# Reordering a few vector, scalar and cast steps in the attention stage of a fused attention / gated MLP / routed attention kernel

## The chip, the cores and the metric

The kernel runs on one core of one Trainium2 chip. The metric is the device time of one execution in microseconds, lower is better; of several executions the median counts. The profile shows the granted clock of TensorE and the span from the first to the last instruction; the device time of an execution is a little longer than its span.

## The reference

Three parts follow each other, for 4 batches of 576 tokens:

```
# 1. windowed causal attention, 8 heads of 64
scores = q @ k.T / 8 + alibi_bias            # key at most 127 behind the query, none ahead
attn   = exp(scores - max);  attn /= sum(attn) + 1e-9
x      = heads side by side of (attn @ v)     # 576 x 512
# 2. gated MLP with a spatial matrix
h = relu(x @ w_in);  u, v = halves of h       # w_in is 512 x 1024
v_n = layer norm of v
gated = u * (w_spatial @ v_n + b_spatial);  x = gated @ w_out
# 3. four attention experts (q, k, v of 64), causal, top 2 of 4 by a gate, summed
```

Only the first part's schedule is touched by the change. Its arithmetic stays as it is.

## The kernel before

The program is written engine by engine: each engine has one instruction stream in program order, and every hand-over is a semaphore. No planner orders the work; the order is the order of the calls in `row(b, ...)` of each engine. `row` is called for batches 0 to 3; in batch 0 `first` is true, and the weights are rounded there beside the attention.

Products that need more than the fast matmul format's precision are made of three matmuls: an operand is split into a rounded part ("hi") and what the rounding lost ("lo"). For w_in, ScalarE makes hi (`high_w_in`, L665 to L668) and VectorE makes lo (`low_w_in`, L989 to L993), one 128x512 block (half, k) at a time, in batch 0 only. Half 1 is the v half, which `v_product` uses first.

The first stage handles a batch in 20 groups g = 0 to 19. A group is two heads of a tile of 128 queries (the last tile has 64 queries, and there two heads share one square). Ten steps m = 0 to 9 of two groups each drive the loops of all engines. A group passes through:

- TensorE `scores1` (L1373 to L1400): q times k into PSUM, two groups at a time.
- VectorE `bias1` (L931 to L945): adds the bias and writes to `ring` in SBUF, with the minimum of the negated row, two instructions (one for each head) of 128x256.
- VectorE `join1` (L947 to L954), called a minimum below: the elementwise minimum of the two key blocks of a row, which turns two blocks of 128 keys into one. A query sees each of the two blocks at complementary positions only.
- ScalarE `exp1` (L644 to L654): the exponential with the row's sum, one instruction and one read of the sum for each head; it waits for the join of its own group.
- VectorE `reciprocal1` (L956 to L963): adds the epsilon to the sums and takes the reciprocal, two small instructions; it waits for the exponentials of its own group. The title of the change calls this step "sums".
- GpSimd `scale1` (L533 to L540): scales the two squares by the reciprocals; it waits for `reciprocal1`.
- TensorE `transpose1` (L1436 to L1442): transposes the scaled squares into PSUM; it waits for `scale1`.
- ScalarE `copy_pt1` (L690 to L698): copies the transposed squares of both groups of a step to `pt` in SBUF (in steps 0 and 1 of the first group only).
- VectorE `copy_pt1_second` (L1017 to L1033): from step 2 on, multiplies this copy by a triangular mask of ones into a second plane of `pt` (L1030, the "masked product"); in steps 0 and 1 it copies the second group's squares (L1025).
- TensorE `values1` (L1463 to L1491): times v. Its first matmuls use the plane of `copy_pt1`; after the first four of them it waits for `copy_pt1_second`, whose plane the difference of two v tiles (`v_step`) is multiplied with.
- ScalarE `high_x`, VectorE `low_x`: the rounded x and the rest, once for each tile.

TensorE's order in a step is: scores of a later step, the two transposes of this step, half of a `v_product` (x times the v half of w_in, six matmuls of 512 columns), `values1` of this step. Beside the diff, these places matter for following it:

```
646    i = G1[g][0];  if i: act.wait_ge(s1_cb, joined1(b, g))   # exp waits for the join
960    dve.wait_ge(s1_ex, U1 * b + us[-1][0] + 1)               # reciprocal waits for the exps
1085   elif m < ND1 - 3:       # steps 4, 5, 6 (and 3): bias, reciprocal1(b, 2 * m + 3), join,
1094       copy_pt1_second(m)  # ... then the masked product, bias, join, reciprocal
```

The order of VectorE in step 5 is thus: bias 14, reciprocal 13, join 14, masked product, bias 15, join 15, reciprocal 14. The change does not touch it. The SyncE queue only issues loads and stores; the change moves none of them.

Of the kernel before, what the change touches and what calls it, by code (L numbers as in the profile page):

```python
# [130 lines left out]
def build(nc, qT, kT, v, w_in, wsT, bsp, woT, wcat, wo, out):  # L131
    ctx = ExitStack()
    with ctx:
# [42 lines left out]
        at = region(4 * NT * H * D)  # L176
# [4 lines left out]
        at = region(max(4 * SLOTS1 * 2 * P, 4 * KT * CW))  # L181
# [4 lines left out]
        at = region(4 * P3_SLOTS * S)  # L186
# [5 lines left out]
        at = region(4 * 2 * 512)  # L192
        pt = sb("pt", [P, 2, 512], F32, at)
        pt_hi = sb("pt_hi", [P, 2, 512], F32R, at)
        at = region(8 * KT * S)
# [9 lines left out]
        at = region(8 * NT * DM)  # L205
# [4 lines left out]
        at = region(4 * 4 * DM)  # L210
# [432 lines left out]
        def _(act):  # L643
            def exp1(b, g):  # L644

                i = G1[g][0]
                if i:
                    act.wait_ge(s1_cb, joined1(b, g))
                for u, h in units1(g):
                    x = ring[:, u % SLOTS1, 0:P]  # L650
                    if i == 0:
                        act.wait_ge(s1_bi, U1 * b + u + 1)
                    nc.scalar.activation(x, x, ACT.Exp, bias=neg1[:, u % SLOTS1:u % SLOTS1 + 1], scale=-1.0,  # L653
                                         accum_out=sum1[:, i % 2, h:h + 1]).then_inc(s1_ex, 1)  # L654
# [34 lines left out]
            def row(b, first, more):  # L689
# [48 lines left out]
                for m in range(ND1):  # L738
                    if m % 2 == 0 and m >= 2:
                        high_x(m // 2 - 1)  # L740
                    if m == 0 and not first:
                        copy_pt1(0)
                        exp1(b, 4)
                        copy_out(b - 1, NT - 1)
                    elif m == 2:
                        copy_pt1(2)
                        for g in (6, 7, 8):
                            exp1(b, g)
                    else:
                        if 2 * m + 3 < NG1 - 1:  # L750
                            exp1(b, 2 * m + 3)
                        copy_pt1(m)
                        if 2 * m + 4 < NG1 and m != 1:
                            exp1(b, 2 * m + 4)
                    if m == ND1 - 3:
                        exp1(b, NG1 - 1)
                    if first and m % 2 and m < ND1 - 1:
                        negate_v(m // 2)
                    for half, at in W_IN_AT.items():
                        for k in range(KT):  # L760
                            if first and at[k] == m:
                                high_w_in(half, k)
                    n = m - first
                    if n % 2 and 3 <= n < ND1 - 1:
                        relu_v((n - 3) // 2)
                    if first:
                        for t in WS_AT.get(m, ()):
                            high_w_spatial(t)
# [161 lines left out]
        def _(dve):  # L930
            def bias1(b, g):  # L931

                qb = ORDER1[G1[g][0]]
                w, c0 = width1(qb), (P if qb == 0 else 0)
                m = g // 2
                at = w * (g % 4 if together(b, m) else g % 2)
                dve.wait_ge(s1_sc, ND1 * b + (m | 1 if together(b, m) else m) + 1)
                for n, (u, h) in enumerate(units1(g)):
                    if qb < NT - 1:
                        scores, table = bank[:, s1_banks(b, g // 2)[n], at:at + w], bias[:, h, c0:c0 + w]  # L940
                    else:
                        scores, table = bank[:, S1_BANKS[g % 2], w * (m % 2):w * (m % 2) + w], bias_last[:, h // 2, :]
                    nc.vector.tensor_tensor_reduce(out=ring[:, u % SLOTS1, 0:w], in0=scores, in1=table, scale=-SCALE,  # L943
                                                   scalar=3.0e38, op0=ALU.add, op1=ALU.min,
                                                   accum_out=neg1[:, u % SLOTS1:u % SLOTS1 + 1]).then_inc(s1_bi, 1)  # L945

            def join1(b, g):  # L947

                if g >= NG1 or G1[g][0] == 0:
                    return  # L950
                n = P if G1[g][0] < NT - 1 else LAST
                dve.wait_ge(s1_bi, U1 * b + units1(g)[-1][0] + 1)
                x = ring[:, slots1(g), :]
                nc.vector.tensor_tensor(x[:, :, 0:n], x[:, :, 0:n], x[:, :, P:P + n], ALU.min).then_inc(s1_cb, 1)  # L954

            def reciprocal1(b, g):  # L956

                us = units1(g)
                at = (slice(0, P), G1[g][0] % 2, slice(us[0][1], us[-1][1] + 1))
                dve.wait_ge(s1_ex, U1 * b + us[-1][0] + 1)  # L960
                nc.vector.tensor_scalar(den1[at], sum1[at], EPS_SUM, None, ALU.add).then_inc(s1_dn, 1)
                dve.wait_ge(s1_dn, NG1 * b + g + 1)
                nc.vector.reciprocal(r1[at], den1[at]).then_inc(s1_rc, 1)  # L963
# [52 lines left out]
            def row(b, first, more):  # L1016
                def copy_pt1_second(m):  # L1017
                    n = 2 * columns1(2 * m)
                    if m:
                        dve.wait_ge(s1_pv, NG1 * b + 2 * m)  # L1020
                    if m < 2:
                        if first:
                            return
                        dve.wait_ge(s1_t, NG1 * b + 2 * m + 2)
                        nc.vector.tensor_copy(pt[:, 0, 2 * P:4 * P], bank[:, 3, 0:2 * P]).then_inc(s1_h2, 1)  # L1025
                        return
                    if m == 2 and first:
                        dve.wait_ge(s_diag, 2)
                    dve.wait_ge(s1_h, ND1 * b + m + 1)
                    nc.vector.tensor_tensor(pt[:, 1, 0:n].rearrange("p (h r) -> p h r", h=4),  # L1030
                                            pt[:, 0, 0:n].rearrange("p (h r) -> p h r", h=4),
                                            diag[:, 0:n // 4].unsqueeze(1).to_broadcast([P, 4, n // 4]), ALU.mult
                                            ).then_inc(s1_h2, 1)  # L1033
# [28 lines left out]
                for m in range(ND1):  # L1062
                    if m % 2 == 0 and m >= 2:
                        low_x(m // 2 - 1)
                    if m == 0 and not first:
                        copy_pt1_second(0)
                        join1(b, 5)
                        reciprocal1(b, 3)
                        reciprocal1(b, 4)
                    elif m == 1:  # L1070
                        copy_pt1_second(1)
                        reciprocal1(b, 5)
                        bias1(b, 6)
                        bias1(b, 7)
                        join1(b, 6)
                    elif m == 2:
                        copy_pt1_second(2)
                        join1(b, 7)
                        bias1(b, 8)
                        reciprocal1(b, 6)  # L1080
                        bias1(b, 9)
                        reciprocal1(b, 7)
                        join1(b, 8)
                        join1(b, 9)
                    elif m < ND1 - 3:
                        bias1(b, 2 * m + 4)
                        if m == 3:
                            reciprocal1(b, 8)
                        else:
                            reciprocal1(b, 2 * m + 3)  # L1090
                        join1(b, 2 * m + 4)
                        if m == 3:
                            reciprocal1(b, 9)
                        copy_pt1_second(m)
                        bias1(b, 2 * m + 5)
                        join1(b, 2 * m + 5)
                        reciprocal1(b, 2 * m + 4)
                    elif m == ND1 - 3:
                        bias1(b, NG1 - 2)
                        bias1(b, NG1 - 1)  # L1100
                        reciprocal1(b, NG1 - 3)
                        join1(b, NG1 - 2)
                        join1(b, NG1 - 1)
                        copy_pt1_second(m)
                        reciprocal1(b, NG1 - 2)
                        reciprocal1(b, NG1 - 1)
                    else:
                        copy_pt1_second(m)
                    for half, at in W_IN_AT.items():
                        for k in range(KT):  # L1110
                            if first and at[k] == m and half:
                                low_w_in(half, k)
# [665 lines left out]
```

## Time and profile before

| what | value |
|---|---|
| median of 3 runs | 488.56 us (488.44 to 489.31) |
| the profiled execution's own time | 489.27 us |
| its span | 487.4 us |
| mean granted TensorE clock | 0.996 |
| TensorE matmul busy | 475.3 us (98%) |
| VectorE busy | 317.8 us (65%) |
| ScalarE busy | 272.9 us (56%) |
| GpSimd busy | 202.9 us (42%) |

The first stage of batch 0 lies at about 4 to 48 us of the span, that of batch 1 at about 144 to 180, of batch 2 at 257 to 293, of batch 3 at 371 to 406. Between them lie the matmuls of parts 2 and 3. A busy row is the share of the span in which the engine had an instruction in work; for TensorE matmuls overlap, so that small stalls hardly show in its busy time. They show as a bracket at the row behind the stall: how long the engine sat idle, and what released it.

### The profile page before, as it was taken

The numbers are of one execution on the slowest core, as the hardware profiler recorded it, in microseconds if no ns is written. First come the engines' busy times: TensorE is split into PE (matmuls) and PEld (weight loads), VectorE is DVE, ScalarE is ACT, GpSimd is POOL, SyncE is SP. The second block draws the span as 40 slices with busy tenths as digits, with TensorE's granted clock in tenths as the row PEclk, the third lists the DMA queues.
The fourth block names the chain that finished last, engine by engine and source line by source line (L and its number), as shares of the span: only waits on it lengthen the run. The fifth ranks groups of instructions, "written<-read, shape, count | busy, mean of one in ns | idle before, by whom it ended". The sixth has DMA issues, their size and how long they took to land.

```text
span 487.4 us, 10761 instructions
## 1 busy us (share of the span) xinstructions
PE 475.3 (98%) x3858; PEld 408.5 (84%) x3858; DVE 317.8 (65%) x1247; ACT 272.9 (56%) x827; POOL 202.9 (42%) x373
## 2 busy tenths in 40 slices
PE   8799999999999999999999999999999999999996
PEld 5577998999776789999876689999877679999974
DVE  7886775367778855337778855436777875235783
ACT  6776572346676644245766745334776663335663
POOL 4361614523434418742244525760343443461431
PEclk9899999999999999999999999999999999999999
DMA  7919420004110081002311073002301000000111
GB/s 230 326 64 245 179 86 1 1 1 135 46 33 23 13 240 42 1 0 53 107 34 44 1 196 98 1 1 48 101 32 56 0 1 2 2 1 12 38 45 54
DMA packets 33512, 31.64 MB, mean 65 GB/s; under 512 B 6002, under 2 KB 24434, under 8 KB 33460
## 3 DMA queue, kind: packets, MB, share of 16 engines
q1 hardware_dynamic: 33460, 30.97, 21.2%
q8 instruction: 30, 0.49, 0.4%
q14 instruction: 22, 0.18, 0.1%
HBM read 23.88 MB, written 4.72 MB: 59 GB/s over the span
## 4 chain that ended last, share of the span: by engine, by line
PE 66%; DVE 17%; ACT 11%; issue 4%; POOL 1%; DVEq 0%
PE bank L1412 14%; PE bank L1414 14%; PE bank L1413 14%; ACT p L830 7%; PE bank L1399 5%; PE bank L1483 5%; DVE ring L943 4%; PE bank L1441 3%; DVE p L1194 2%; PE bank L1690 2%; PE bank L1668 2%; PE bank L1418 2%; DVE ring L954 2%; PE bank L1419 1%; DVE pt L1030 1%
## 5 line engine op out<-in xcount | busy, mean ns | idle before, releaser
L539 POOL TENSOR_SCALAR ring<-ring,r 128x128 f32<-128x128 f32 x144 | 60.2, 430 | 86.1 <-DVE r L963 85.8
L625 POOL TENSOR_SCALAR p<-p,r,wgt 128x128 f32<-128x128 f32 (+3 forms) x64 | 38.3, 610 | 93.3 <-DVE wgt_last L1241 50.0
L653 ACT ACTIVATE ring<-ring,neg 128x128 f32<-128x128 f32 x144 | 56.7, 396 | 21.3 <-DVE ring L954 18.1
L830 ACT ACTIVATE p<-p,neg 128x128 f32<-128x128 f32 (+4 forms) x72 | 41.6, 579 | 29.6 <-DVE neg L1194 29.6
L943 DVE CUSTOM_DVE_ANT_0 ring<-bank,bias 128x256 f32<-128x256 f32 (+1 forms) x128 | 43.5, 384 | 2.3 <-PE bank L1399 2.0
L589 POOL TENSOR_TENSOR g_lo<-uT,g_hi 128x288 fp32r<-128x288 f32 x32 | 25.2, 814 | 36.4 <-ACT g_hi L796 20.4
L1412 PE MATMUL bank<-g_hi,w_c_hi 128*128 128x288 f32 x128 | 38.6, 301 | 0.2
L1412 PE MATMUL bank<-x_hi,w_in_hi 128*128 128x288 f32 x128 | 38.2, 298 | 0.0
L1412 PE MATMUL bank<-w_spatial_hi,vn_hi 128*128 128x288 f32 x128 | 37.8, 295 | 0.0
L1414 PE MATMUL bank<-x_hi,w_in_lo 128*128 128x288 f32 x128 | 37.7, 295 | 0.0
L1414 PE MATMUL bank<-w_spatial_hi,vn_lo 128*128 128x288 f32 x128 | 37.7, 294 | 0.0
L1413 PE MATMUL bank<-w_spatial_lo,vn_hi 128*128 128x288 f32 x128 | 37.7, 294 | 0.0
L1413 PE MATMUL bank<-x_lo,w_in_hi 128*128 128x288 f32 x128 | 37.7, 294 | 0.0
L1414 PE MATMUL bank<-g_hi,w_c_lo 128*128 128x288 f32 x128 | 37.7, 294 | 0.0
L1413 PE MATMUL bank<-g_lo,w_c_hi 128*128 128x288 f32 x128 | 37.5, 293 | 0.0
L1399 PE MATMUL bank<-k,q 64*128 64x256 f32 (+2 forms) x320 | 36.8, 367 | 0.0
L1194 DVE CUSTOM_DVE_ANT_0 p<-bank,causal_masks 128x128 f32<-128x128 f32 (+4 forms) x72 | 34.3, 513 | 1.6 <-PE bank L1653 1.4
L1483 PE MATMUL bank<-pt,v_in 128*64 128x128 f32 (+1 forms) x384 | 33.0, 274 | 0.6 <-ACT pt L695 0.6
L796 ACT CAST g_hi<-uT 128x288 fp32r<-128x288 f32 x32 | 12.9, 432 | 35.7 <-DVE uT L1173 35.7
L1483 PEld LDWEIGHTS bank<-pt,v_in 128*64 128x64 f32 x384 | 20.5, 137 | 14.1 <-issue 12.2
L1399 PEld LDWEIGHTS bank<-k,q 64*128 64x128 f32 (+1 forms) x320 | 26.1, 182 | 6.7 <-issue 4.1
L1173 DVE TENSOR_TENSOR uT<-bank,uT 128x288 f32<-128x288 f32 x32 | 13.5, 454 | 27.7 <-PE bank L1596 27.7
(193 smaller groups left out, 1449.0 us busy)
## 6 DMA issues: line engine op xcount, KB each, us to landing
v_in<-v SPq DMA_DIRECT2D x16, 256.0 KB, 4.0
out<-o_sb SPq DMA_DIRECT2D x16, 256.0 KB, 2.0
q<-qT SPq DMA_DIRECT2D x15, 256.0 KB, 4.6
k<-kT SPq DMA_DIRECT2D x15, 256.0 KB, 5.1
v_minus_v_of_tile_above<-v SPq DMA_DIRECT2D x9, 256.0 KB, 3.8
w_in_raw<-w_in SPq DMA_DIRECT2D x4, 512.0 KB, 6.2
w_cat_raw<-wcat SPq DMA_DIRECT2D x1, 1544.0 KB, 6.8
w_spatial_raw<-wsT SPq DMA_DIRECT2D x1, 1152.0 KB, 9.3
```

The lines of the kernel that those rows point to most:

```text
L539: last = nc.gpsimd.tensor_scalar(p, p, r1[:, i % 2, h:h + 1], 0.0, ALU.mult, ALU.add)
L589: nc.gpsimd.tensor_tensor(g_lo[:, dt, c], uT[:, dt, c], g_hi[:, dt, c].bitcast(F32), ALU.subtract).then_inc(s2_gl, 1)
L625: nc.gpsimd.tensor_scalar(p, p, r3[:, i % 2, e:e + 1], by, ALU.mult, ALU.mult).then_inc(s3_sd, 1)
L653: nc.scalar.activation(x, x, ACT.Exp, bias=neg1[:, u % SLOTS1:u % SLOTS1 + 1], scale=-1.0, accum_out=sum1[:, i % 2, h:h + 1]).then_inc(s1_ ...
L830: nc.scalar.activation(p, p, ACT.Exp, bias=neg3[:, w % 4:w % 4 + 1], scale=-1.0, accum_out=sum3[:, i % 2, es[0]:es[0] + 1]).then_inc(s3_ex, 1)
L943: nc.vector.tensor_tensor_reduce(out=ring[:, u % SLOTS1, 0:w], in0=scores, in1=table, scale=-SCALE, scalar=3.0e38, op0=ALU.add, op1=ALU.mi ...
L1194: nc.vector.tensor_tensor_reduce(out=p3[:, w % P3_SLOTS, 0:n], in0=scored3(w), in1=mask3(w), scale=-1.0, scalar=3.0e38, op0=ALU.add, op1=A ...
L1399: last = nc.tensor.matmul(to, q1[half, k, tok(qb)], k1[half, k, k0:k0 + w], start=True, stop=True)
L1412: nc.tensor.matmul(to, hi_l, hi_r, start=first, stop=False)
L1413: nc.tensor.matmul(to, hi_l, lo_r, start=False, stop=False)
L1414: return nc.tensor.matmul(to, lo_l, hi_r, start=False, stop=last)
L1483: last = nc.tensor.matmul(bank[D * (h % 2):D * (h % 2) + D, x_bank(i), at:at + r], values[:, h, :], pt[:, part, c:c + r], start=start, sto ...
```

## The change

It moves calls within ScalarE's and VectorE's streams; no instruction is added or taken away.

- ScalarE, step 2: in batch 0 the first two roundings of w_in (half 1, k = 0 and 1) come between the exponentials of groups 7 and 8 rather than behind group 8.
- ScalarE, step 5, in all batches: the copy of the transposed squares comes ahead of the exponentials of group 13 rather than behind them.
- VectorE, step 0, batches 1 to 3: the reciprocal of group 3 comes ahead of the join of group 5.
- VectorE, step 2, in all batches: the reciprocal of group 6 comes ahead of the bias of group 8, and that of group 7 ahead of the bias of group 9.

```diff
@@ scalar, row @@
                     elif m == 2:
                         copy_pt1(2)
-                        for g in (6, 7, 8):
-                            exp1(b, g)
+                        exp1(b, 6)
+                        exp1(b, 7)
+                        if first:
+                            high_w_in(1, 0)
+                            high_w_in(1, 1)
+                        exp1(b, 8)
+                    elif m == 5:
+                        copy_pt1(5)
+                        exp1(b, 13)
+                        exp1(b, 14)
                     else:
                         if 2 * m + 3 < NG1 - 1:
                             exp1(b, 2 * m + 3)
...
-                            if first and at[k] == m:
+                            if first and at[k] == m and m != 2:
                                 high_w_in(half, k)
@@ vector, row @@
                     if m == 0 and not first:
                         copy_pt1_second(0)
+                        reciprocal1(b, 3)
                         join1(b, 5)
-                        reciprocal1(b, 3)
                         reciprocal1(b, 4)
...
                     elif m == 2:
                         copy_pt1_second(2)
                         join1(b, 7)
+                        reciprocal1(b, 6)
                         bias1(b, 8)
-                        reciprocal1(b, 6)
+                        reciprocal1(b, 7)
                         bias1(b, 9)
-                        reciprocal1(b, 7)
                         join1(b, 8)
                         join1(b, 9)
```

## Rows read from the trace of the kernel before

**Rows 1.** The page: busy time, share of the span, instructions of each engine.

```profile
PE 475.3 (98%) x3858; PEld 408.5 (84%) x3858; DVE 317.8 (65%) x1247; ACT 272.9 (56%) x827; POOL 202.9 (42%) x373
```

**Rows 2.** TensorE's waits, first stages of batches 0, 1, 2: us, times, longest.

```profile
PE bank L1441 <- POOL ring L539: 1.3, 2, 0.9
...
PE bank L1441 <- POOL ring L539: 0.7, 2, 0.5
...
PE bank L1483 <- DVE pt L1030: 0.4, 1, 0.4
```

**Rows 3.** Timeline, batch 1, step 5: start, duration, engine, instruction, idle before.

```profile
163.63 0.40 ACT L653 ACTIVATE ring<-ring,neg 128x128 f32<-128x128 f32 x1 [1.20 <-DVE ring L954]
...
164.41 0.56 ACT L695 COPY pt<-bank 128x512 f32<-128x512 f32 x1
...
164.54 0.17 DVE L961 TENSOR_SCALAR den<-sum 128x2 f32<-128x2 f32 x1
...
164.83 0.40 DVE L954 TENSOR_TENSOR ring<-ring 128x256 f32<-128x256 f32 x1
165.15 0.68 DVE L1030 TENSOR_TENSOR pt<-pt,keys_up_to_query 128x512 f32<-128x512 f32 x1
...
163.39 0.66 PE L1441 MATMUL bank<-ident,ring 128*128 128x128 f32 x4
...
165.89 0.44 PE L1483 MATMUL bank<-pt,v_minus_v_of_tile_above 128*64 128x128 f32 x4
```

**Rows 4.** Timeline, batch 1, step 4: the transposes, the copy and an exponential.

```profile
160.38 0.66 PE L1441 MATMUL bank<-ident,ring 128*128 128x128 f32 x4
...
161.07 0.59 ACT L695 COPY pt<-bank 128x512 f32<-128x512 f32 x1 [1.15 <-PE bank L1441]
...
161.55 0.41 ACT L653 ACTIVATE ring<-ring,neg 128x128 f32<-128x128 f32 x1
```

**Rows 5.** Timeline, batch 0, step 5: TensorE's transposes and the first value products.

```profile
30.41 0.66 PE L1441 MATMUL bank<-ident,ring 128*128 128x128 f32 x4
...
32.37 0.74 PE L1483 MATMUL bank<-pt,v_in 128*64 128x128 f32 x8
```

**Rows 6.** Timeline, batch 1, steps 0 and 1; last, a later scaling behind a join.

```profile
145.86 0.42 DVE L954 TENSOR_TENSOR ring<-ring 128x256 f32<-128x256 f32 x1
146.19 0.16 DVE L961 TENSOR_SCALAR den<-sum 128x2 f32<-128x2 f32 x1
...
146.65 1.42 POOL L539 TENSOR_SCALAR ring<-ring,r 128x128 f32<-128x128 f32 x4 [1.37 <-DVE r L963]
...
147.42 0.44 PE L1441 MATMUL bank<-ident,ring 128*128 128x128 f32 x2 [0.22 <-POOL ring L539]
...
160.93 0.81 POOL L539 TENSOR_SCALAR ring<-ring,r 128x128 f32<-128x128 f32 x2 [1.11 <-DVE r L963]
```

**Rows 7.** Timeline, batch 1, steps 2 and 3.

```profile
153.87 0.24 DVE L961 TENSOR_SCALAR den<-sum 128x2 f32<-128x2 f32 x1
...
154.67 0.40 ACT L653 ACTIVATE ring<-ring,neg 128x128 f32<-128x128 f32 x1 [1.45 <-DVE ring L954]
...
155.53 0.44 PE L1441 MATMUL bank<-ident,ring 128*128 128x128 f32 x2 [0.52 <-POOL ring L539]
...
157.64 0.20 PEld L1483 LDWEIGHTS bank<-pt,v_minus_v_of_tile_above 128*64 128x64 f32 x4 [0.15 <-DVE pt L1030]
```

**Rows 8.** Timeline, batch 0, steps 2 and 3.

```profile
19.79 1.29 DVE L992 TENSOR_TENSOR w_in_lo<-w_in_raw,w_in_hi 128x512 fp32r<-128x512 f32 x2 [1.12 <-ACT w_in_hi L668]
...
22.57 0.69 DVE L1030 TENSOR_TENSOR pt<-pt,keys_up_to_query 128x512 f32<-128x512 f32 x1
...
20.63 0.76 PE L1412 MATMUL bank<-w_in_hi,x_hi 128*128 128x512 f32 x1 [0.96 <-DVE w_in_lo L992]
...
23.46 0.79 PE L1483 MATMUL bank<-pt,v_in 128*64 128x128 f32 x8
```

**Rows 9.** Stretch table, batch 0, 21 to 22 us: PE, PEld, DVE, ACT, POOL busy, granted clock.

```profile
21.00:22.00 1.00, 1.00 (x3) 0.76 (x3) 0.96 (x8) 0.53 (x2) 0.00 (x0) 0.50 1.05 380
```

## The prediction

> **What bounds the kernel now.** I read the busy shares first: TensorE has matmuls in work for 98% of the span [rows 1], and the longest stretches of the chain that ended last are its matmuls. So a microsecond by which another engine holds TensorE up is lost for good, and any other idle time costs nothing. The change sits in the first stage, so I read next what TensorE waited for in the first stage of each batch [rows 2]. In batch 0 it waits 1.3 us for scaled squares, and 1.0 us for the low part of w_in [rows 8]; in batches 1 to 3 it waits 0.7 us for scaled squares, at two places, and in batch 2 another 0.4 us for the masked product. That is nearly all that a better order could give: 2.3 us in batch 0 and about 0.7 in each other one. Last I read the timeline around each moved call, engine by engine, to see who is late by how much and who queues behind it.
>
> **The change part by part.** Times are of batch 1 unless said; batches 2 and 3 repeat them.
>
> *Step 5, the copy ahead of exponentials 13.* Before, exponentials 13 start at 163.63 as their join is done, and the reciprocal of group 13 starts at 164.54 behind them, 0.91 us later; then come join 14 (164.83) and the masked product (165.15), and TensorE's next value products start at 165.89 [rows 3]. The transposes start at 163.39, and a copy that truly waits for its transposes starts 0.69 us after their start (160.38 to 161.07) [rows 4]. So the copy, put first, would start at 163.39 + 0.69 = 164.08, only 0.33 us sooner than the 164.41 of before, and ScalarE, idle for 1.20 us ahead of 163.63, still has to sit there until the transposes are through. The exponentials follow it. From the copy's start to the next exponential are 0.48 us (161.07 to 161.55) [rows 4]. Exponentials 13 then start at 164.56 and their sums are there at 165.47. On VectorE the reciprocal of group 13 stands ahead of join 14 and the masked product, and the change leaves that so. It blocks VectorE until 165.47; the join follows at 165.76, the masked product at 166.08, and with its 0.68 and a hand-over of 0.06 TensorE goes on at 166.82 instead of 165.89: **+0.92 us**. The copy's 0.33 us buys nothing, because TensorE's first four value products, which need it, stand behind a v_product that is still running then. What is queued behind the waiting reciprocal is late by the same 0.93: join 14, exponentials 14, bias 15. They feed work that TensorE reaches later still, so they add nothing. In batch 2 the masked product was already late by 0.4 [rows 2], from an idle time of VectorE that a wait of 0.93 would cover: there the loss is 0.92 − 0.4 = **+0.5**. Batch 3 is as batch 1. In batch 0 the transposes start at 30.41 [rows 5]; the same chain (0.69 + 0.48 + 0.91 + 0.29 + 0.32 + 0.68 + 0.06 = 3.43) ends at 33.83, where TensorE needed the product at about 32.67, four short matmuls behind 32.37: **+1.15**. Sum of step 5: 0.92 + 0.5 + 0.92 + 1.15 = **+3.5 us**.
>
> *Step 0, the reciprocal of group 3 ahead of join 5 (batches 1 to 3).* The join holds VectorE for 0.33 us (145.86 to 146.19). The reciprocals then release the scaling at 146.65, and the transposes of group 3 wait 0.22 us idle and start at 147.42 [rows 6]. With the reciprocal first the scaling starts 0.33 us sooner. Join 5's own exponentials stand behind those of group 4 and a copy of an output tile on ScalarE, so nobody misses the join. But the scaling now runs beside the join. A scaling of two squares alone is half of the four's 1.42, 0.71; one that starts just behind a join's start took 0.81 [rows 6], 0.1 more. I take 0.33 − 0.1 = 0.23 less (bounds 0.1 and 0.34). All that follows up to step 2 hangs on TensorE, so it passes on: **−0.7** in three batches.
>
> Rows show the 0.1. The Trainium skill, "SBUF — State Buffer", Who interferes with whom, states it as a lock: a VectorE operation with two SBUF inputs and a GpSimd operation that reads SBUF exclude each other, and the second to issue waits until the first ends. By that rule the delay here would be the rest of the join, about 0.1 us, the same; in step 2, where the scaling would start first, the join would wait instead, which would make the sum some 0.6 us larger than by the rows.
>
> *Step 2, the two reciprocals ahead of two biases.* Scaling 7 starts about 0.7 us sooner, and the wait of 0.52 us at 155.53 goes [rows 7]. But what is late next is not changed: exponentials 8 wait 1.45 us for join 8, which stands behind the same VectorE work as before, and start at 154.67, since the biases and reciprocals are only permuted (the reciprocal at 153.87 ends its pair as the joins begin). Behind exponentials 8 and 9 comes the copy of step 3, then the masked product, for which the weights of TensorE's value products wait at 157.64 [rows 7]. TensorE gets to its v_product 0.7 us sooner and then waits 0.7 us for the masked product. I cost it at +0.05 in each of batches 1 to 3, between −0.1 (the reciprocal at 153.87 took 0.24 where others take 0.17) and +0.2 (the moved scaling, at 153.7 to 154.4, may hold join 8 up): **+0.15**.
>
> *Step 2 in batch 0, with the roundings.* ScalarE is idle ahead of exponentials 8 for 1.45 us in batch 1 [rows 7], and the same number stands in batch 0. The two casts take 1.1 us and fit. Then VectorE need not wait the 1.12 us for them and goes straight from its joins to the low parts, at 18.67 and not at 19.79 [rows 8]: it runs 1.12 us ahead. TensorE's v_product starts at 19.5 instead of 20.63, the masked product at 21.45 instead of 22.57. In that v_product TensorE's clock was granted at half, 1.2 GHz [rows 9], behind stalls of 1.3 and 1.0 us in sum; with about 1.1 us of stall left rather than 2.3 I expect it to stay at 2.4. The value products then are bound by the masked product: 21.45 + 0.69 + 0.05 = 22.2 for their second part, before at about 23.8 (23.46 and four matmuls at half clock). **−1.6** (bounds −0.3, if the clock falls later and the value products run at half, and −1.7). The casts read w_in some 2 us sooner than before; no row shows them waiting for its load, and if it were not there yet, the gain would shrink towards that lower bound.
>
> Sum: +3.5 − 0.7 + 0.15 − 1.6 = **+1.35, say +1.4 us**. It is made against the profiled execution (489.27, 487.4 its span and 1.9 around it), which stands 0.7 above the median; on the median it gives 488.56 + 1.4 = 490.0. Differences under 0.2% (0.98 us) a measurement of this kernel can hardly tell from none.
>
> **The rivals.** *Faster: the late masked product is not on the path.* If in step 5 TensorE had something between the first four value products and the rest, or if exponentials 13 did not delay VectorE's queue, the 3.5 us would fall away and −0.7 + 0.15 − 1.6 = −2.2 would stay: 486.4. It decides at 165.9 in batch 1: VectorE may be late until then and no later. For it speaks that step 5 was quiet before, with no wait of TensorE in [rows 2] but batch 2's; against it, that this was so by 0.05 us only: the masked product's end (165.83) and TensorE's start (165.89) touch. 0.12.
>
> *No measurable change: the same mechanisms, with sizes that meet.* If the copy gives way sooner, step 5 costs 0.7 in each batch, and the moved reciprocals give their bounds: 3 × 0.7 + 0.9 − 1.0 − 1.7 = +0.3: 488.9. 0.30.
>
> *Much slower: the clock.* A stall of about 1.2 us in step 5 adds to the quiet of the engine. If the clock fell there as at 21 us [rows 9], the next v_product would take the 2.8 us of the one from 20.63 to 23.46 [rows 8], which at full clock I estimate at half of that: +1.4 in each batch, 5.6 in all: 495.6. Against it: in batch 0 2.3 us of stalls stood ahead of the fall, twice as much. 0.05.
>
> **How the numbers follow.** The forecast has 0.53, with its own range from 489.5 to 491.2. The range 488.2 to 491.2 takes in most of the case without change and leaves out the faster case and the clock, 0.17, with some of the tails. Slower by over 0.2% is the forecast and the clock, less the forecast's low edge: 0.56; faster 0.13; within 0.31.
>
> **What would show it.** In the changed kernel TensorE's waits for the masked product (L1030) in each first stage should grow to about 1 us in step 5, with VectorE idle 0.9 us ahead of a reciprocal step released by ScalarE; the 0.22 and 0.52 us waits for the scaling should shrink to 0.1 and nothing, and a wait for the masked product should stand in step 3. In batch 0 the wait for w_in's low part should stay near 0.9 us, at 19.5, with the clock at 1.0. The forecast is wrong if value products of step 5 start within 2.6 us of their transposes.

## The result and the profile after

The changed kernel is slower: 491.28 us (490.59 to 491.88, 10 runs) against 489.19 us (488.33 to 490.75, 10 runs) of the kernel before, ratio 1.0034 with a 95% interval of 1.0019 to 1.0049. That is +0.9 to +2.4 us, +1.7 in the middle. The kernel before came out 0.6 us higher here than in the three runs shown ahead of the prediction; on their 488.56 the ratio makes 490.2, where 490.0 was forecast. The median as measured, 491.28, stands just above the forecast's own range, whose upper end was 491.2. The profiled execution took 491.3 us, its span is 489.6, 2.2 more than before.

Busy times are the same to 1 us, as they should be where no instruction is added. From the page of the changed kernel:

```profile
span 489.6 us, 10761 instructions
PE 474.4 (97%) x3858; PEld 407.9 (83%) x3858; DVE 318.0 (65%) x1247; ACT 272.9 (56%) x827; POOL 202.5 (41%) x373
```

Line numbers behind L747 are larger than before by 8, behind the change on VectorE too (in the versions further below the same lines stand 4 to 16 higher than before): L1038 is the masked product (L1030 before), L1449 the transposes, L1407 the scores, L1420 to L1422 the product of three, L1491 the value products. What TensorE waited for in the first stages of batches 0, 1 and 2 (us in total, times, longest), to be held against [rows 2]:

```profile
PE bank L1491 <- DVE pt L1038: 1.7, 2, 1.0
PE bank L1420 <- DVE w_in_lo L1000: 0.9, 1, 0.9
...
PE bank L1449 <- POOL ring L539: 0.4, 1, 0.4
...
PE bank L1491 <- DVE pt L1038: 1.4, 2, 1.0
...
PE bank L1491 <- DVE pt L1038: 1.6, 2, 1.2
```

The waits for the scaling are nearly gone, and waits for the masked product, twice in each batch, stand in their place. The longest of each batch is the one of step 5. Its timeline in batch 1, to be held against [rows 3]:

```profile
163.93 0.59 ACT L695 COPY pt<-bank 128x512 f32<-128x512 f32 x1 [1.63 <-PE bank L1449]
164.41 0.41 ACT L653 ACTIVATE ring<-ring,neg 128x128 f32<-128x128 f32 x1
...
165.32 0.17 DVE L969 TENSOR_SCALAR den<-sum 128x2 f32<-128x2 f32 x1 [0.91 <-ACT ring L653]
...
165.61 0.40 DVE L962 TENSOR_TENSOR ring<-ring 128x256 f32<-128x256 f32 x1
165.93 0.68 DVE L1038 TENSOR_TENSOR pt<-pt,keys_up_to_query 128x512 f32<-128x512 f32 x1
...
163.23 0.66 PE L1449 MATMUL bank<-ident,ring 128*128 128x128 f32 x4
...
166.67 0.44 PE L1491 MATMUL bank<-pt,v_minus_v_of_tile_above 128*64 128x128 f32 x4 [1.03 <-DVE pt L1038]
```

The copy waits 1.63 us for the transposes, the exponentials follow it, VectorE sits idle for 0.91 us in front of the reciprocal, and the masked product behind it comes late. From the transposes to the second part of the value products it is 3.44 us now; it was 2.50.

The whole stage can be read as a ledger. I take the start of TensorE's scores as marks (scores of steps 2, 4 and 6, and in step 0 from the first value products to the scores of step 1), so that what happened earlier falls out. Microseconds, from the timelines:

| stretch | batch | before | changed | difference |
|---|---|---|---|---|
| step 0, value products to scores | 1, 2, 3 | 1.61 each | 1.37, 1.38, 1.38 | −0.7 in all |
| scores of step 2 to those of step 4 | 0 | 11.03 | 9.41 | −1.62 |
| same | 1, 2, 3 | 8.42, 8.41, 8.41 | 8.50, 8.50, 8.49 | +0.25 in all |
| scores of step 4 to those of step 6 (holds step 5) | 0 | 8.86 | 10.04 | +1.18 |
| same | 1, 2, 3 | 8.24, 8.58, 8.25 | 9.17, 9.34, 9.17 | +0.93, +0.76, +0.92 |

The sum is +1.7 us. Of the rest of the 2.2 us between the spans, 0.45 was there before the first changed instruction: the first transposes of batch 0 start at 9.20 instead of 8.75. The 11.03 of batch 0 was taken with TensorE's clock at half for part of the stretch [rows 9]; what that is worth comes further below.

### The profile page after: what moved, and what is told of

It reads as the page before. It is cut to its first block, busy times and chain, and to the rows that moved or that the text cites. A ratio compares the mean times of both kernels' runs of the same rounds, so it can differ in the third digit from the quotient of the medians.

```text
span 489.6 us, 10761 instructions
## 1 busy us (share of the span) xinstructions
PE 474.4 (97%) x3858; PEld 407.9 (83%) x3858; DVE 318.0 (65%) x1247; ACT 272.9 (56%) x827; POOL 202.5 (41%) x373
## 4 chain that ended last, share of the span: by engine, by line
PE 68%; DVE 15%; ACT 13%; issue 4%; DVEq 0%
PE bank L1420 14%; PE bank L1422 14%; PE bank L1421 14%; ACT p L838 7%; PE bank L1491 6%; PE bank L1407 5%; PE bank L1449 3%; PE bank L1698 3%; DVE ring L951 3%; DVE p L1202 2%; PE bank L1676 2%; ACT ring L653 2%; DVE pt L1038 2%; PE bank L1426 2%; DVE ring L962 2%
## 5 line engine op out<-in xcount | busy, mean ns | idle before, releaser
L539 POOL TENSOR_SCALAR ring<-ring,r 128x128 f32<-128x128 f32 x144 | 58.9, 422 | 89.1 <-DVE r L971 88.9
L1420 PE MATMUL bank<-g_hi,w_c_hi 128*128 128x288 f32 x128 | 38.6, 302 | 0.3
L1420 PE MATMUL bank<-x_hi,w_in_hi 128*128 128x288 f32 x128 | 38.2, 298 | 0.0
L1420 PE MATMUL bank<-w_spatial_hi,vn_hi 128*128 128x288 f32 x128 | 37.8, 295 | 0.0
L1422 PE MATMUL bank<-x_hi,w_in_lo 128*128 128x288 f32 x128 | 37.7, 294 | 0.0
L1422 PE MATMUL bank<-w_spatial_hi,vn_lo 128*128 128x288 f32 x128 | 37.7, 294 | 0.0
L1422 PE MATMUL bank<-g_hi,w_c_lo 128*128 128x288 f32 x128 | 37.7, 294 | 0.0
L1407 PE MATMUL bank<-k,q 64*128 64x256 f32 (+2 forms) x320 | 37.0, 367 | 0.0
L1491 PE MATMUL bank<-pt,v_in 128*64 128x128 f32 (+1 forms) x384 | 33.3, 273 | 3.2 <-DVE pt L1038 1.7
L1491 PEld LDWEIGHTS bank<-pt,v_in 128*64 128x64 f32 x384 | 20.4, 136 | 17.1 <-issue 11.4
L695 ACT COPY pt<-bank 128x512 f32<-128x512 f32 (+1 forms) x40 | 19.9, 497 | 23.6 <-PE bank L1449 23.6
L1407 PEld LDWEIGHTS bank<-k,q 64*128 64x128 f32 (+1 forms) x320 | 26.1, 182 | 6.9 <-issue 4.1
```

Of the source, the lines that this page charges most:

```text
L539: last = nc.gpsimd.tensor_scalar(p, p, r1[:, i % 2, h:h + 1], 0.0, ALU.mult, ALU.add)
L1407: last = nc.tensor.matmul(to, q1[half, k, tok(qb)], k1[half, k, k0:k0 + w], start=True, stop=True)
L1420: nc.tensor.matmul(to, hi_l, hi_r, start=first, stop=False)
L1422: return nc.tensor.matmul(to, lo_l, hi_r, start=False, stop=last)
L1491: last = nc.tensor.matmul(bank[D * (h % 2):D * (h % 2) + D, x_bank(i), at:at + r], values[:, h, :], pt[:, part, c:c + r], start=start, sto ...
```

## The experiments

**Only the copy of step 5.** On the kernel before:

```diff
                             exp1(b, g)
+                    elif m == 5:
+                        copy_pt1(5)
+                        exp1(b, 13)
+                        exp1(b, 14)
                     else:
```

> The kernel before with one part of the change, the copy of step 5 ahead of exponentials 13 and 14. Theory (the chain copy, exponentials 13, reciprocal 13, join 14, masked product on in-order queues): TensorE waits about 1 us more for the masked product in step 5 of every batch, 1.18 + 0.93 + 0.76 + 0.92 as in the changed kernel's ledger, in all +3.8 us on the kernel before. Rival (the stall only shows because the other moves bring TensorE forward): clearly less, about +1.7 us or under. Rival (the slowdown does not come from this part): no change.

Measured: 493.32 us, ratio 1.0083 (1.0069 to 1.0097), +4.1 us. The stretches with step 5 take 10.03, 9.16, 9.34 and 9.17 us, +3.8 in all, to 0.01 those of the changed kernel. The whole loss and more is this one move; the other moves neither cause nor ease it.

**All but the copy of step 5.** The changed kernel without those four lines.

> The changed kernel with the step 5 move of the copy undone. Theory: what is left are the gains, -1.6 in batch 0 from the roundings, 3 x -0.23 from the reciprocal of step 0, 3 x +0.08 from the reciprocals of step 2, in all -2.1 us on the kernel before, and TensorE's wait for the masked product in step 5 is gone (but 0.4 us in batch 2). Rival (the reciprocals of step 2 cost as much as they give, because TensorE waits for the masked product in step 3 too): -2.1 us all the same, but if something in the rest of the change loses time, 0 or above.

Measured: 487.72 us, ratio 0.9966 (0.9954 to 0.9978), −1.7 us; the −2.1 expected lies inside the interval (−2.2 to −1.1). The step 5 stretches are back at 8.81, 8.25, 8.54 and 8.26. The rest of the change is a gain. In batch 1 TensorE's waits now are:

```profile
PE bank L1487 <- DVE pt L1034: 0.4, 1, 0.4
PE bank L1487 <- ACT pt L695: 0.3, 1, 0.3
```

That is step 3: the wait for scaling 7 [rows 7] has become one for the copy and the masked product.

**The copy first, and the masked product ahead of the reciprocal.** On the changed kernel:

```diff
                         bias1(b, 2 * m + 4)
+                        if m == 5:
+                            copy_pt1_second(m)
                         if m == 3:
                             reciprocal1(b, 8)
...
-                        copy_pt1_second(m)
+                        if m != 5:
+                            copy_pt1_second(m)
```

> The changed kernel, the copy of step 5 still ahead of exponentials 13, but VectorE's masked product of step 5 moved ahead of reciprocal 13 and join 14. Theory (TensorE only waits because the masked product is queued behind a reciprocal that waits for the late exponentials): the masked product ends at 1.9 us behind the start of the transposes, before TensorE needs it, the wait in step 5 vanishes in all batches, batch 2's old 0.4 us too; -2.5 us on the kernel before. Rival (the late exponentials 13 themselves cost, through scaling 13 and the transposes of step 6): the wait moves to those transposes and the kernel stays 1 to 2 us slower than before.

Measured: 488.69 us, ratio 0.9990 (0.9980 to 1.0001), no difference that can be told from the kernel before. By the two ratios, 0.9990 and 1.0034, it takes 2.1 us less than the changed kernel. But by the medians it takes 1.0 us more than the one without the copy move, where my theory had it 0.4 faster. In batch 1:

```profile
164.75 0.69 DVE L1038 TENSOR_TENSOR pt<-pt,keys_up_to_query 128x512 f32<-128x512 f32 x1 [0.20 <-ACT pt L695]
165.46 0.17 DVE L969 TENSOR_SCALAR den<-sum 128x2 f32<-128x2 f32 x1
...
166.40 0.42 DVE L951 CUSTOM_DVE_ANT_0 ring<-bank,bias 128x256 f32<-128x256 f32 x1
...
165.60 0.39 PE L1494 MATMUL bank<-pt,v_minus_v_of_tile_above 128*64 128x128 f32 x4
...
166.98 1.52 PE L1410 MATMUL bank<-k,q 64*64 64x192 f32 x16 [0.55 <-DVE neg L951]
```

The masked product now is early and the value products run without a gap: the chain of the theory holds. But the wait was handed on. The scores of step 6 overwrite the banks that bias 15 reads, and bias 15 still stands behind the late reciprocal. In the changed kernel this was hidden behind the value products, which were as late. Neither theory named this wait; the rival looked for it at the transposes.

**The same pair of moves in step 3 as well.** On top of the last one, the copy ahead of exponentials 9 and 10, and the masked product ahead of reciprocal 9:

```diff
-                    elif m == 5:
-                        copy_pt1(5)
-                        exp1(b, 13)
-                        exp1(b, 14)
+                    elif m in (3, 5):
+                        copy_pt1(m)
+                        exp1(b, 2 * m + 3)
+                        exp1(b, 2 * m + 4)
...
+                        if m != 5:
+                            copy_pt1_second(m)
                         if m == 3:
                             reciprocal1(b, 9)
```

> As the one with the masked product first in step 5, and the same pair of moves in step 3: the copy ahead of exponentials 9 and 10, the masked product ahead of reciprocal 9. Theory (what held TensorE in step 3 after the change is the chain exponentials 9, copy, reciprocal 9, masked product): the wait of 0.4 to 0.7 us for the masked product in step 3 goes, -0.7 us in each of batches 1 to 3 and -0.3 in batch 0 more, in all -4.9 us on the kernel before. Rival (exponentials 9 and 10 and scaling 9, now later, hold up the transposes of step 4): the wait moves to the transposes and the time stays at -2.5 us.

Measured: 486.23 us, ratio 0.9940 (0.9928 to 0.9952), −2.9 us. It stands 2.4 us under the one before it, as expected, with the base off by what that one was off. The stretches from step 2 to step 4 take 9.13, 7.80, 7.79 and 7.80 us, against 9.41 and 8.49 to 8.51.

**Step 3 with the copy of step 5 undone.**

```diff
-                    elif m == 5:
-                        copy_pt1(5)
-                        exp1(b, 13)
-                        exp1(b, 14)
+                    elif m == 3:
+                        copy_pt1(3)
+                        exp1(b, 9)
+                        exp1(b, 10)
...
+                        copy_pt1_second(m)
                         if m == 3:
                             reciprocal1(b, 9)
-                        copy_pt1_second(m)
```

> The changed kernel with the step 5 move undone, and instead in step 3 the copy ahead of exponentials 9 and 10 and the masked product ahead of reciprocal 9. Theory: the two parts add, the kernel without the copy move (-1.7 us on the kernel before) and what step 3 gave on top of the one with the masked product first (-2.5 us): -4.1 us on the kernel before, no wait for the masked product in step 3 and none of the waits for bias 15 (0.5 us) in step 5. Rival (step 3's gain came from elsewhere): -1.7 us.

Measured: 484.96 us, ratio 0.9912 (0.9899 to 0.9925), −4.3 us. This version beats both kernels. Its batch 1:

```profile
152.70 0.66 PE L1449 MATMUL bank<-ident,ring 128*128 128x128 f32 x4
...
154.67 0.44 PE L1491 MATMUL bank<-pt,v_in 128*64 128x128 f32 x4
155.14 0.44 PE L1491 MATMUL bank<-pt,v_minus_v_of_tile_above 128*64 128x128 f32 x4
...
155.94 2.00 PE L1407 MATMUL bank<-k,q 64*128 64x256 f32 x16
```

The copy and the masked product of step 3 here, and in the kernel without the copy of step 5 (batch 1; transposes at 154.18 there):

```profile
153.67 0.56 ACT L695 COPY pt<-bank 128x512 f32<-128x512 f32 x1
154.40 0.68 DVE L1038 TENSOR_TENSOR pt<-pt,keys_up_to_query 128x512 f32<-128x512 f32 x1
...
155.92 0.56 ACT L695 COPY pt<-bank 128x512 f32<-128x512 f32 x1
156.59 0.69 DVE L1034 TENSOR_TENSOR pt<-pt,keys_up_to_query 128x512 f32<-128x512 f32 x1 [0.16 <-ACT pt L695]
```

The copy starts 0.97 us behind the transposes instead of 1.74, the masked product 1.70 instead of 2.41. The pair of moves gains 0.7 us in step 3; in step 5 the same pair costs 0.3 in batches 1 and 3, 0.2 in batch 0 and nothing in batch 2 (stretches of 8.54, 8.53, 8.99 and 8.53 with the masked product first, against 8.25, 8.26, 8.81 and 8.54), and the copy alone costs 0.9. The difference is in what ScalarE does meanwhile. In step 3 it has exponentials 8 to do until the transposes are through, and the copy starts with no idle time ahead of it. In step 5 it has nothing, and the copy makes it wait. Neither half of the pair was run alone in step 3. The last row says that the masked product alone could have given little there, since it was released by the copy (ACT pt), not by the reciprocal ahead of it.

**Step 3 alone, without the reciprocals of step 2.** The same diff on the kernel before.

> The kernel before with the moves of step 3 alone: the copy ahead of exponentials 9 and 10, the masked product ahead of reciprocal 9. Theory (two waits stand one behind the other in steps 2 and 3: transposes 7 for scaling 7, and the value products for the copy and the masked product; either alone hides the other): the copy then waits for transposes 7, which come as late as before, and starts at about the time it had, so the gain is 0.1 us or less in each batch, within 0.3 us of the kernel before. Rival (the two gains simply add): the 2.3 us by which copy_in_step3 beat no_copy.

Measured: 489.18 us, ratio 0.9995 (0.9982 to 1.0008), no difference. In batch 1 the copy now has to wait for transposes 7, and they for scaling 7:

```profile
156.22 0.44 PE L1445 MATMUL bank<-ident,ring 128*128 128x128 f32 x2 [0.53 <-POOL ring L539]
...
156.69 0.59 ACT L695 COPY pt<-bank 128x512 f32<-128x512 f32 x1 [0.45 <-PE bank L1445]
```

The moves of step 3 alone give 0.14 us in batch 1 (8.28 against 8.42), the reciprocals of step 2 alone cost 0.08, and both give 0.64 (7.78). Two waits stood one behind the other, and each hid the other.

**The copy first in steps 3 and 5, bias 15 early.** The last attempt to make the copy of step 5 pay; VectorE in step 5 as bias 14, masked product, join 14, bias 15, reciprocal 13, join 15, reciprocal 14.

```diff
+                    elif m == 5:
+                        bias1(b, 14)
+                        copy_pt1_second(m)
+                        join1(b, 14)
+                        bias1(b, 15)
+                        reciprocal1(b, 13)
+                        join1(b, 15)
+                        reciprocal1(b, 14)
                     elif m < ND1 - 3:
```

> The copy ahead of the exponentials in both steps 3 and 5, and in step 5 VectorE in the order bias 14, masked product, join 14, bias 15, reciprocal 13, join 15, reciprocal 14. Theory (with the masked product first the scores of step 6 only wait because bias 15 stands behind reciprocal 13, which waits for the late exponentials 13): the wait of the scores shrinks from 0.5 us to 0.1, TensorE loses nothing for the masked product, and the copy's move is worth 0.2 us in each of batches 1 to 3: -4.5 us on the kernel before. Rival (exponentials 13 and 14, 0.9 us late, then hold up scaling 13 or the rounding of x): a wait for GpSimd or for x's low part shows in step 6, -3 us or less.

Measured: 485.10 us, ratio 0.9916 (0.9901 to 0.9931), the same as without the copy of step 5. In batch 1:

```profile
PE bank L1415 <- DVE neg L951: 0.2, 1, 0.2
```

The wait of the scores shrank from 0.55 to 0.2 us, not 0.1. The stretch with step 5 takes 8.16 us in batch 1 against 8.25, and 0.1 of that is lost again two steps later (the transposes of step 7 start 1.12 us behind the value products instead of 1.02). Batch 3 repeats this. Only batch 2 keeps a gain: 8.17 against 8.58, and 0.34 of it is still there at the last transposes of its first stage. So even with everything behind it put right, the moves in step 5 are worth 0.3 us in one batch, too little for the timing to show, and not the 0.2 in each of batches 1 to 3 that I expected.

**Only the two roundings.** On the kernel before, the ScalarE lines of step 2 alone.

```diff
-                        for g in (6, 7, 8):
-                            exp1(b, g)
+                        exp1(b, 6)
+                        exp1(b, 7)
+                        if first:
+                            high_w_in(1, 0)
+                            high_w_in(1, 1)
+                        exp1(b, 8)
```

> The kernel before with the one move of the two w_in roundings ahead of exponentials 8. Theory: only batch 0 changes; VectorE is 1.1 us ahead from the low parts on, and with TensorE's clock at 2.4 GHz in the v_product of step 3 that is all: -1.1 us; -1.6 us only against an execution in which the clock was granted at half there, as in the profiled execution before. Rival (the gain of batch 0 needs the moved reciprocals too, since the transposes of group 7 wait for scaling 7): the v_product starts no sooner than at 20.3 us and the gain is under 0.5 us.

Measured: 489.28 us, ratio 0.9982 (0.9969 to 0.9995), −0.9 us. The stretch from step 2 to step 4 takes 9.42 us in batch 0, as in the changed kernel (9.41): in this execution, whose clock stayed at full, the reciprocals add nothing in that batch. The rival was right on the place and wrong on the price: the v_product did start as late as 20.41, because of scaling 7.

```profile
20.22 0.44 PE L1445 MATMUL bank<-ident,ring 128*128 128x128 f32 x2 [1.89 <-POOL ring L539]
20.41 0.48 PE L1416 MATMUL bank<-w_in_hi,x_hi 128*128 128x512 f32 x1
...
17.97 0.74 DVE L958 TENSOR_TENSOR ring<-ring 128x256 f32<-128x256 f32 x2
18.63 1.38 DVE L996 TENSOR_TENSOR w_in_lo<-w_in_raw,w_in_hi 128x512 fp32r<-128x512 f32 x2
...
21.49 0.69 DVE L1034 TENSOR_TENSOR pt<-pt,keys_up_to_query 128x512 f32<-128x512 f32 x1
...
18.15 2.02 POOL L539 TENSOR_SCALAR ring<-ring,r 128x128 f32<-128x128 f32 x2 [0.32 <-DVE r L967]
```

It cost nothing, since the second four value products wait for the masked product in any case: it starts at 21.49, 7.43 us behind the scores of step 2, as in the changed kernel, and ends at 22.18.

**Only the two reciprocals of step 2**, and **only the reciprocal of step 0**, each on the kernel before, with one execution each.

```diff
                         join1(b, 7)
+                        reciprocal1(b, 6)
                         bias1(b, 8)
-                        reciprocal1(b, 6)
+                        reciprocal1(b, 7)
                         bias1(b, 9)
-                        reciprocal1(b, 7)
```

> The kernel before with only the two reciprocals of step 2 moved. Theory: the waits of 0.5 us for scaling 7 turn into waits for the masked product in step 3, in each of batches 1 to 3 the scores of step 4 start 0.08 us later relative to the scores of step 2, because join 8 and 9 run beside scaling 7; in batch 0 TensorE waits for the low part of w_in as long as before. In all +0.2 us. Rival (a full lock between join and scaling): +0.2 us in each batch, +0.6 in all.

```diff
+                        reciprocal1(b, 3)
                         join1(b, 5)
-                        reciprocal1(b, 3)
```

> The kernel before with only reciprocal 3 ahead of join 5. Theory: scaling 3 starts 0.34 us sooner and takes 0.1 longer beside the join, TensorE's scores of step 1 start 0.23 us sooner in each of batches 1 to 3 relative to the first transposes of the batch, -0.7 us in all. Rival (the transposes are bound by TensorE itself once the wait of 0.22 us goes): -0.2 us times 3 at most, and the lead is lost again by step 3.

Single runs of 489.99 and 487.75 us say little; the stretches do. With the reciprocals of step 2, batches 1 to 3 take 8.50, 8.50 and 8.49 us from step 2 to step 4, +0.08 each; batch 0 takes 11.24, +0.2, which I had not expected. The clock was at half there between 24 and 25 us too (0.67 in the mean; 1.00 in the kernel before), so that it still held when the value products began at 23.94. With the reciprocal of step 0, the way from the value products to the scores of step 1 falls from 1.61 to 1.37, 1.36 and 1.37, and the 0.24 is kept in step 3 (8.41 from step 2 to step 4).

## Why the prediction was right, and where it was off

**Step 5: right, term by term.** +0.92, +0.5, +0.92 and +1.15 were forecast, the ledger shows +0.93, +0.76, +0.92 and +1.18. The copy starts 0.70 us behind its transposes (0.69 was taken), the exponentials 0.48 behind that. The cause is shown: the copy alone gives the whole loss, undoing it takes all of it away. The one term that was mis-sized is batch 2, forecast at +0.5 and measured at +0.76. I had the lateness of 0.4 us down as an idle time of VectorE that the new wait would cover. In the changed kernel VectorE waits the same 0.91 us there, and then the masked product takes 0.81 instead of 0.68 us:

```profile
279.25 0.17 DVE L969 TENSOR_SCALAR den<-sum 128x2 f32<-128x2 f32 x1 [0.91 <-ACT ring L653]
...
279.90 0.81 DVE L1038 TENSOR_TENSOR pt<-pt,keys_up_to_query 128x512 f32<-128x512 f32 x1
```

So part of the oddity of that batch stayed. The trace of the kernel before tells what it is. The first square of scaling 13 in batch 1, then join 14, that square and the masked product in batch 2:

```profile
165.00 0.99 POOL L539 TENSOR_SCALAR ring<-ring,r 128x128 f32<-128x128 f32 x1 [0.32 <-DVE r L963]
...
277.98 0.40 DVE L954 TENSOR_TENSOR ring<-ring 128x256 f32<-128x256 f32 x1
278.16 0.47 POOL L539 TENSOR_SCALAR ring<-ring,r 128x128 f32<-128x128 f32 x1 [0.32 <-DVE r L963]
278.61 0.72 DVE L1030 TENSOR_TENSOR pt<-pt,keys_up_to_query 128x512 f32<-128x512 f32 x1 [0.22 <-issue]
```

One square takes 0.37 us on GpSimd when VectorE leaves it alone. In batch 1 it took 0.99 and ended at 165.99, 0.16 behind the masked product's end [rows 3]: GpSimd was held up. In batch 2 it took 0.47, and the masked product started only as it ended (278.63), with 0.22 us idle that no semaphore ended: VectorE was held up. So the 0.4 us stand behind the reciprocal, not ahead of it, and no wait at the reciprocal can cover them. Moving the masked product away from the scaling does: with it ahead of the reciprocal the stretch with step 5 takes 8.53 us in batch 2 and 8.54 in batch 1. Why the scaling comes first in batch 2 and not in batches 1 and 3 no run tells.

**"They feed work that TensorE reaches later still, so they add nothing": right only as long as the value products are late too.** Bias 15 feeds the banks of the very next scores. With the value products on time, these waited 0.55 us. The prediction's sum is not touched, but whoever mends the kernel by that sentence, as I did, ends 1.0 us above the kernel without the copy's move instead of below it.

**Step 0: right.** −0.7 forecast, −0.7 in the ledger. Scalings 3 and 4 took 1.52 us together, where they took 1.42 [rows 6]:

```profile
146.33 1.52 POOL L539 TENSOR_SCALAR ring<-ring,r 128x128 f32<-128x128 f32 x4 [1.03 <-DVE r L971]
```

That is the 0.1 taken for the scaling beside the join. Join 5 stood in these rows:

```profile
146.15 0.41 DVE L962 TENSOR_TENSOR ring<-ring 128x256 f32<-128x256 f32 x1
```

By the rule of the Trainium skill, "SBUF — State Buffer", Who interferes with whom, the scaling would wait for the join's end at 146.56, 0.23 us; the prediction had put that at about 0.1. The trace shows 0.10 of it, so here the measurement decides.

**Step 2 in batches 1 to 3: right.** +0.05 each forecast, +0.08 measured. The 0.7 us that TensorE waits in step 3 are there too, 0.32 of them for the copy and 0.36 for the masked product. The moved scaling does reach into the joins:

```profile
153.51 0.72 POOL L539 TENSOR_SCALAR ring<-ring,r 128x128 f32<-128x128 f32 x2 [0.32 <-DVE r L971]
...
154.00 0.83 DVE L962 TENSOR_TENSOR ring<-ring 128x256 f32<-128x256 f32 x2
...
154.53 0.40 ACT L653 ACTIVATE ring<-ring,neg 128x128 f32<-128x128 f32 x1 [1.53 <-DVE ring L962]
...
157.50 0.44 PE L1491 MATMUL bank<-pt,v_minus_v_of_tile_above 128*64 128x128 f32 x4 [0.36 <-DVE pt L1038]
```

The two joins take 0.83 instead of 0.74 us, and exponentials 8 start 0.53 behind the joins' start, not 0.44. By the same section of the Trainium skill whole instructions shut each other out, and the first join would have waited for the scaling's end at 154.23, 0.23 later. The trace shows 0.09 of it; here too the measurement decides.

**Step 2 in batch 0: right, with one thing unsaid.** The ledger has −1.62 for −1.6. The forecast put about 0.5 us of it to TensorE's clock, which "I expect to stay at 2.4". It did. But the kernel before does not always run that stretch with the clock at half. With nothing moved ahead of step 5, the copy-only kernel had the same stalls in steps 2 and 3 (1.3 and 1.0 us), and its clock stayed at full. Stretch table, 20 to 23 us, of the copy-only kernel (the last figures are the granted clock, the DMA share and GB/s):

```profile
20.00:23.00 3.00, 2.08 (x12) 1.33 (x14) 2.93 (x13) 2.12 (x10) 1.25 (x2) 1.00 1.05 388
```

and of the kernel before:

```profile
20.00:23.00 3.00, 2.37 (x6) 1.82 (x6) 2.93 (x12) 2.12 (x9) 0.86 (x2) 0.56 1.01 363
```

The copy-only kernel took 10.54 us from step 2 to step 4 in batch 0, not 11.03. So the roundings are worth 1.1 us against an execution whose clock stays up and 1.6 against one in which it falls; timed, −0.9 us (−1.5 to −0.2).

The mean clocks of all executions tell how often it falls. The three profiled ones with a mean of 0.996 or 0.997 all show the fall at 20 us, and none of those with 0.999 or 1.0 does. By that sign the clock fell in 32 of the 54 executions of the kernel before that the experiments have (median 489.7 us, against 488.6 of the other 22), in 3 of 6 with the copy alone, in 8 of 12 with step 3 alone and in 7 of 12 with the roundings alone. It fell in none of the 47 executions of the six versions that have both the roundings and the reciprocals of step 2, the changed kernel among them. So the reciprocals do add something in batch 0 that the stretches of one profiled execution do not show: only together with them do the roundings keep the clock up every time. The stalls for scaling 7 and for w_in's low part are 0.4 and 0.9 us then, where the roundings alone had 1.9 for the scaling. Against executions of the kernel before whose clock stays up, the changed kernel loses 2.2 us by the ledger.

**The rivals.** The late masked product was on the path, as its 0.05 us of slack had said. The clock did not fall in step 5, with stalls of 1.0 to 1.2 us: it is at 1.00 in all first stages of the changed kernel, and the mean is 0.999 or 1.0 in all ten of its executions.

## What to carry to other kernels

Putting an instruction first on an in-order engine is free only if its input is there by the time the engine would reach it: here the copy put first, with the masked product moved up behind it, gained 0.7 us where ScalarE was busy until the transposes were through and lost 0.3 where it was idle, and 0.9 without the masked product's move. Follow the instructions that it was put in front of to what waits for them, across the engines and up to the bottleneck, and also to the one behind (bias 15), which becomes visible once the first wait is mended. Where two waits stand one behind the other, trying each fix alone shows nothing or a small loss; the timeline behind the vanished wait tells what the second one is.

## What the runs showed of the hardware that I had not expected

- A GpSimd scaling of two 128x128 squares took 2.02 us instead of 0.72 while VectorE ran two joins and two differences of 128x512, all with both inputs in SBUF, one behind the other (the kernel with the roundings alone, from 18.15). The first square took 0.72 and ended 0.16 behind the second join, the second square took 1.32 (row below) and ended 0.16 behind the second difference. So each square was held over two instructions of VectorE. The Trainium skill, "SBUF — State Buffer", Who interferes with whom, has the second to issue wait until the first finishes; here it waited for more than one.

```profile
18.85 1.32 POOL L539 TENSOR_SCALAR ring<-ring,r 128x128 f32<-128x128 f32 x1
```

- TensorE's clock at 20 us was granted at half in the profiled executions of the kernel before and of step 3 alone, and at full in those of the copy alone and of step 0 alone. The four have the same order of work up to there; only the start is shifted, with the scores of step 2 at 14.02, 14.62, 13.62 and 13.89 us. What decides it in one execution no run here tells.
- The start of the kernel moves the whole execution. In the kernel without the copy of step 5 TensorE waited for a load of k, its warming matmuls behind that ran longer, and the scores of step 1 started at 9.08 us; in the changed kernel they started at 8.13. All that follows is shifted by such amounts, which is as much as the changes under test, so the stretches between marks tell more than the spans:

```profile
5.49 1.22 PE L1403 MATMUL bank<-k,q 64*128 64x128 f32 x8 [0.33 <-DMA k<-kT]
6.65 2.50 PE L1412 MATMUL bank<-pt_hi 128*128 128x512 f32 x5
9.08 1.28 PE L1403 MATMUL bank<-k,q 64*128 64x256 f32 x8
```
